# Weighing the values ahead of the transposes of q and k and the cluster products, in a clustered attention and feed-forward kernel

## The reference, cut to what matters

```python
mask = q_assign[:, :, :, None] == k_assign[:, :, None, :]   # nearest of 16 centroids, per head
scores = scale * np.matmul(q, k.transpose(0, 1, 3, 2))      # 2 batches x 8 heads, 768 x 768
scores = np.where(mask, scores, -1000000000.0)
scores = scores - np.max(scores, axis=-1, keepdims=True)
attn = np.exp(scores)
attn = attn / (np.sum(attn, axis=-1, keepdims=True) + 1e-09)
return np.matmul(attn, v)
...
a = x @ w1                       # x: 1536 x 512, the attention's output
b = x @ w2
x = ((a * b) @ w3) @ w_out
h = x @ w_in
g = np.maximum(h, 0.0) + alpha * np.minimum(h, 0.0)
out = g @ w_out2
```

## Time and profile before

| | |
|---|---|
| median of 3 runs | 748.01 us |
| the profiled execution | 747.64 us |
| its span (first to last instruction) | 745.8 us |
| TensorE matmuls | 739.0 us busy, 99% |
| TensorE weight loads | 641.6 us busy, 86% |
| VectorE | 411.8 us busy, 55% |
| ScalarE | 311.6 us busy, 42% |
| GpSimd | 179.5 us busy, 24% |
| granted TensorE clock | 0.999 of full speed, on average |

### The profile page before, as it was taken

One profiled execution on the slowest core, in us unless ns is written; L12 is line 12 of the kernel. 1 busy time (PEld: TensorE's weight loads), 2 busy tenths in 40 slices (PEclk: granted clock), 3 DMA queues, 4 the chain that ended last, 5 costly groups with the idle time before them and its releaser, 6 DMA issues.

```text
span 745.8 us, 10690 instructions
## 1 busy us (share of the span) xinstructions
PE 739.0 (99%) x3792; PEld 641.6 (86%) x3792; DVE 411.8 (55%) x632; ACT 311.6 (42%) x623; POOL 179.5 (24%) x211
## 2 busy tenths in 40 slices
PE   8999999999999999999999999999999999999998
PEld 6888999999999998888888888888888888888886
DVE  4435999999999984721311432575434333343432
ACT  5235988988988884311211422432012111121111
POOL 2141566866865893500000000000000000000000
PEclk9999999999999999999999999999999999999999
DMA  9636366566566233300000022140001000010001
GB/s 293 195 94 144 78 152 155 124 146 154 127 146 153 65 84 92 98 29 1 1 0 1 20 93 85 57 130 11 1 0 57 1 0 1 1 56 1 1 0 57
DMA packets 65371, 54.17 MB, mean 73 GB/s; under 512 B 32032, under 2 KB 54576, under 8 KB 65328
## 3 DMA queue, kind: packets, MB, share of 16 engines
q1 hardware_dynamic: 65328, 53.59, 27.9%
HBM read 31.50 MB, written 3.19 MB: 47 GB/s over the span
## 4 chain that ended last, share of the span: by engine, by line
PE 97%; DVE 1%; DMA 1%; ACT 1%; issue 0%; SPq 0%; DVEq 0%; ACTq 0%
PE slot L625 63%; PE acc L625 24%; PE slot L689 9%; PE acc L638 1%; PE slot L737 1%; DMA early<-in_moe_w_out 1%; DVE xl L1163 0%; DVE xl L1145 0%; ACT xh L938 0%; ACT xh L945 0%; DVE abx L1283 0%; DVE ab L1279 0%; ACT abx L1055 0%; ACT asb L1041 0%; ACT ost L1108 0%
## 5 line engine op out<-in xcount | busy, mean ns | idle before, releaser
L625 PE MATMUL slot<-xh,w 128*128 128x512 f32 x768 | 248.0, 389 | 0.0
L625 PEld LDWEIGHTS slot<-xh,w 128*128 128x128 f32 x768 | 144.1, 188 | 29.8
L625 PE MATMUL slot<-xl,w 128*128 128x512 f32 x384 | 149.4, 389 | 0.0
L1101 ACT CAST gh<-gf 128x512 fp32r<-128x512 f32 x48 | 29.9, 623 | 203.2 <-PE acc L625 186.0
L1206 DVE TENSOR_TENSOR pl<-slot,ph 128x384 fp32r<-128x384 f32 x192 | 97.6, 549 | 8.5 <-ACT ph L973 8.2
L1200 DVE TENSOR_REDUCE nm<-slot 128x1 f32<-128x768 f32 x96 | 91.4, 952 | 15.4 <-PE slot L625 13.8
L973 ACT CAST ph<-slot 128x384 fp32r<-128x384 f32 x192 | 83.5, 489 | 34.3 <-PE slot L689 33.8
L965 ACT ACTIVATE pf<-slot,nm 128x768 f32<-128x768 f32 x96 | 88.4, 921 | 4.6 <-DVE nm L1200 4.5
L625 PEld LDWEIGHTS slot<-xl,w 128*128 128x128 f32 x384 | 72.1, 188 | 15.0
L625 PE MATMUL slot<-k,q 80*128 80x384 f32 (+1 forms) x384 | 82.9, 337 | 0.0
L1329 DVE TENSOR_TENSOR gl<-gf,gh 128x512 fp32r<-128x512 f32 x48 | 33.2, 692 | 89.9 <-ACT gh L1101 89.9
(11 more groups left out here) (121 smaller groups left out, 1012.0 us busy)
## 6 DMA issues: line engine op xcount, KB each, us to landing
stage<-in_moe_w SPq DMA_DIRECT2D x16, 256.0 KB, 3.5
stage<-in_moe_w_in SPq DMA_DIRECT2D x16, 256.0 KB, 2.7
stage<-in_moe_w_out SPq DMA_DIRECT2D x16, 256.0 KB, 3.0
stage<-in_moe_w SPq DMA_DIRECT2D x6, 512.0 KB, 4.2
qk<-in_q SPq DMA_DIRECT2D x16, 192.0 KB, 3.9
qk<-in_k SPq DMA_DIRECT2D x16, 192.0 KB, 3.9
vn<-in_v SPq DMA_DIRECT2D x16, 192.0 KB, 3.8
q<-k SPq DMA_DIRECT2D x16, 192.0 KB, 3.8
```

The costliest lines, as they stand in the source:

```text
L625: return nc.tensor.matmul(o, a, b, start=start, stop=stop)
L1101: copy(gh[j % 2][:, :], gf[j % 2][:, :]).then_inc(gh_done, 1)
```

## The change

In TensorE's order within a step, `weigh` now stands ahead of the prepared work and not behind it. No instruction is added or taken away; the orders of VectorE, ScalarE, GpSimd and SyncE are the same.

```diff
@@ -714,13 +714,13 @@
                     score(it, c)
                 if there(c - LT):
                     turn_probabilities(it, c - LT)
+                if there(c - LW):
+                    weigh(it, c - LW)
                 for kind, j, half in prepared(it, c, last):
                     if kind == "turned":
                         turned(it, j, half)
                     elif kind == "cluster":
                         cluster(it, j, half)
-                if there(c - LW):
-                    weigh(it, c - LW)
```

## The result

| | before | after |
|---|---|---|
| median (of the runs compared) | 747.95 us (4 runs, 747.85 to 748.18) | 758.62 us (4 runs, 758.28 to 758.78) |
| the profiled execution | 747.64 us | 758.73 us |
| its span | 745.8 us | 756.9 us |
| granted TensorE clock | 0.999 | 1.0 |

The change makes the kernel slower: the ratio is 1.0142, with a 95% interval of 1.0131 to 1.0154, 10.7 us between the medians. 758.3 was predicted.

What follows compares the result with a forecast made beforehand. TensorE was taken to bound the kernel: 10.0 us of new waits plus 0.3 us over the profiled 747.64 gives 757.9, and 0.37 to the median gives 758.3 us. Its own range was 756 to 762, the wider one 753 to 764.

Steps and rivals of the forecast that it cites:

- What bounds the kernel: Attention, 60 to 296 us: TensorE busy 235.75 of 236.00 us, so every new wait there goes straight into the time.
- The moved work costs nothing: TensorE's order: transposes and cluster matmuls that only change place cost 0.
- ScalarE comes 0.60 us late: In m = 10 operands_hi starts at 167.20, not 166.60, and pushes out_copy from 167.94 to 168.54.
- Place one: m = 11: weigh can start at 169.15 but TensorE arrives at 168.27; new wait 0.88 us.
- Place two: m = 2: weigh can start at 176.25 but TensorE arrives at 175.46; new wait 0.79 us.
- How often: Each of the two waits, in m = 11 and m = 2, occurs six times, once a lap: 10.0 us.
- What is late next: VectorE's maximum and low parts behind a late operands_lo, with 0.1 to 0.2 us left: 0.3 us added in all.
- The VectorE case: Transposes of exponentials in m = 0 and 1 also wait, for pl_done: 5.4 us more, 763.7 us; chance 0.09.
- Half: One of the two places, m = 11 or m = 2, stays covered: 5 us, 753.0 us; chance 0.05.
- no change: TensorE's waits are covered or operands_hi doesn't hold the exponential up: 748.0 us; chance 0.03.
- faster: Earlier pv_done brings out_copy forward, and the 0.13 us waits in m = 5 and 8 vanish: 745.9 us; chance 0.03.
- clock: Twelve gaps of 0.8 us on TensorE bring its clock to 1.2 GHz: at most 57 us, 805; chance 0.02.

Runs made afterwards that it cites:

- run 9: Changed kernel, with ScalarE's out_copy directly behind the casts of the step before only in m = 10 and 1 of the six laps: 747.75 us, ratio 0.9997.
- run 1: Kernel before, with weigh ahead of the prepared work only in m = 0, 1, 3 and 10: 752.98 us, ratio 1.0067.
- run 2: Kernel before, with weigh ahead of the prepared work only in m = 2 and 11: 752.49 us, ratio 1.0061.
- run 4: Kernel before, with weigh ahead of the transposes of q and k only (m = 0, 1, 10, 11): 754.98 us, ratio 1.0095.
- run 5: Kernel before, with weigh ahead of the prepared work only in m = 0 and 3: 748.98 us, ratio 1.0013.
- run 6: Kernel before, with weigh ahead of the prepared work only in m = 1: 749.42 us, ratio 1.0020.
- run 7: Changed kernel, with ScalarE's exponential ahead of operands_hi, its copies of turned q and k: 762.14 us, ratio 1.0190.
- run 10: Kernel before, with ScalarE's out_copy moved from the head of m = 2, 5, 8, 11 to behind the casts of the step before: 754.12 us, ratio 1.0084.
- run 8: Changed kernel, with ScalarE's out_copy moved from the head of m = 2, 5, 8, 11 to behind the casts of the step before: 746.39 us, ratio 0.9982.
- run 11: Kernel before, with ScalarE's out_copy ahead of the exponential only in steps that turn no q and k: 746.49 us, ratio 0.9985.
- run 3: Kernel before, with weigh ahead of the cluster products only (m = 2 and 3): 749.58 us, ratio 1.0022.

## Why the prediction was right

*What bounds the kernel* held: each microsecond of new wait on TensorE stood in the time.

*The moved work costs nothing* held. The order of work by itself made no time: run 9 has the change's whole order on TensorE and the time of before.

*ScalarE comes 0.60 us late* held. In m = 10 the copy of turned q and k started 0.40 us ahead of the next scores (166.60 and 167.00), and now starts 0.28 us behind them (173.11 and 172.83), of which 0.09 is that a matmul behind transposes is shown early. The last of the transposes that began at 172.58 starts at 172.80; the copy starts at 173.11, 0.31 behind it, the number taken from another pair of rows.

*Place one, 0.88 us:* measured 0.87. *Place two, 0.79 us:* measured 0.80 in four laps and 0.89 in two, the upper of my two values for the time from copy to matmul; the prediction had the lower at all six. *How often, six laps:* held. The sum, 10.0 against 10.2 measured.

*What is late next, 0.3 us in all:* this was a guess, and no wait that answers to it was found. The spans of the two profiled executions lie 11.1 us apart, of which 0.5 stand ahead of the first `weigh`, where the two kernels do the same (its six transposes start at 71.22 and 71.71 us), and 10.6 behind it. So 0.4 us are left beside the 10.2 us of waits, less than the runs of one kernel differ (758.28 to 758.78), and their cause stays open. VectorE's lateness did not reach the transposes of exponentials: their waits for its low parts are 1.4 us over six times, as in the trace of before.

*The rivals.* The VectorE case did not come in this kernel, but I judged it by the wrong semaphore. I looked at `pl_done`, and at `prep_free` only for SyncE's queue. In the change that is harmless. In runs 1, 2 and 4, where prepared work still stood at the front of a step, my expectations were 1.7 to 1.9 us short; this wait is 1.5 us of that in runs 1 and 4 and 1.1 us in run 2. Runs 5 and 6 show the size where it stands alone. That it vanishes in the full change is luck of the prediction: it never looked at this wait on TensorE. With the exponential moved (run 7) the ring through VectorE and ScalarE sets the pace of the steps that turn q and k. *Half* and *no change* are ruled out by the timeline; the *faster* rival was right that earlier `pv_done` is worth something, but only once `out_copy` is placed to use it (7.7 us between runs 10 and 8); the 1.4 us by which run 8 beats the kernel before don't come from it (run 11). The *clock* stayed at 1.00 with twelve new gaps of 0.8 to 0.9 us: the rule of the Trainium skill (TensorE: Matmul & The Clock Gate, A second HAM failure mode: psum-queue depth-cycling) did not come into play here.

*What would show it.* The 1.45 and 1.38 us lie in the ranges given. Two signs came out only in part. ScalarE's idle time ahead of `operands_hi` was to be 0.6 us in all turning steps; it is 0.50 and 0.69 in m = 10 and 11 but 0.17 and 0.18 in m = 0 and 1, because there the late copy of the step before has pushed ScalarE's exponential and casts back as well. And the wait of weight loads for L982 was to hold about 10 us, with under 7 as a sign of being wrong. By name it holds 3.2 us, at four places; most of the rest stands under "issue", 7.8 us. The rows of the matmuls name L982 for 3.5 + 2.5 = 6.0 us, ten of the twelve places, and tell of the same waits. By that sign alone the prediction would have been called wrong. The view splits one wait by releaser and by engine and shows less of it than the delay (0.63 us at the matmul where the distances show 0.87), so the sign should have been put on distances.

## What to carry to other kernels

Before moving work on a busy engine, list for each piece who reads its result and what stands behind that reader in its own order: here TensorE lost 0.9 us at a time to a copy that was late only because an unrelated one stood ahead of it. A wait that is covered shows no idle time in a profile, so compare the distance to the releasing instruction with what that release needs elsewhere (0.66 against 0.61 us here), not the idle column. And try the order of the waiting engine together with the order of the one it waits for: the same move cost 10.7 us or gained 7.7 depending on where one copy stood.

## What the runs showed of the hardware that was not expected

From the start of ScalarE's copy to the matmul that it releases it is 0.52 to 0.54 us where that release is the last wait of the matmul alone (189.02 to 189.54 before, 182.54 to 183.07 after, 175.88 to 176.42 in run 3), and 0.60 to 0.64 where a further wait stands between them or, behind the loop, both waits are on the matmul (182.58 to 183.19, 174.47 to 175.07 and 241.69 to 242.32 after, 203.93 to 204.57 in run 3). That these 0.1 us come from the number or place of the waits is read from the order of the program and was not tried by itself.
